# Two transfers under way: pacing GpSimd's row transfers in the first MoE layer

## The reference

```python
def reference(x, h, moe_*, moe2_*):             # cut
    # 1: causal convolution of x (4, 5696, 128) with h (5696, 128) along the sequence, by FFT
    x = irfft(rfft(x, n=2*S) * rfft(h, n=2*S)[None], n=2*S)[:, :S].reshape(22784, 128)
    # 2: MoE layer 1, 8 experts, capacity 22784 / 8 = 2848 tokens each
    logits = x @ w_gate
    for idx in argsort(-logits.flatten()):      # greedy: best (token, expert) pairs first
        tok, e = idx // 8, idx % 8
        if assigned[tok] < 0 and counts[e] < 2848: assigned[tok] = e; counts[e] += 1
    out[mask_e] = relu(x[mask_e] @ w1[e]) @ w2[e]           # 128 -> 1024 -> 128
    # 3: MoE layer 2: expert = argmax of a token's logits, no capacity
    out[mask_e] = gate_w[mask_e] * (relu(x[mask_e] @ w1b[e]) @ w2b[e])
    # gate_w: the softmax weight of the chosen expert
```

## Time and profile before

| What | Value |
|---|---|
| median of three runs | 2315.74 us |
| profiled execution: its own time; its span | 2332.93 us; 2331.1 us |
| mean granted TensorE clock | 0.919 |
| PE, DVE, ACT, POOL busy over the span | 84%, 55%, 41%, 31% |
| 743 to 1712 us (layer 1): PE, DVE, ACT, POOL busy | 781.0, 530.4, 328.1, 425.0 of 969 us |
| the same: granted clock; share of the DMA engines; GB/s | 0.91; 0.12; 35 |
| 1712 to 2331 us (layer 2): PE busy | 606.0 of 619.1 us |
| GpSimd's fetches (line 1650), 192 | median 997 ns, 941 to 2405 |
| GpSimd's sends (line 1659), 192 | median 987 ns, 968 to 1417 |
| PE idle ahead of line 828, for the fetched rows | 20.1 us in 13 places |

### The profile page before, as it was taken

One profiled execution on the slowest core, in us unless ns is written; L12 is line 12 of the kernel. 1 busy time (PEld: TensorE's weight loads), 2 busy tenths in 40 slices (PEclk: granted clock), 3 DMA queues, 4 the chain that ended last, 5 costly groups with the idle time before them and its releaser, 6 DMA issues.

```text
span 2331.1 us, 36413 instructions
## 1 busy us (share of the span) xinstructions
PE 1953.3 (84%) x10729; PEld 1517.2 (65%) x10729; DVE 1288.8 (55%) x4137; ACT 950.9 (41%) x2046; POOL 722.1 (31%) x618
## 2 busy tenths in 40 slices
PE   7886898699723988787878787987959999999998
PEld 3343444355422766565666665765759999999998
DVE  2224777422388675656666665511246666666665
ACT  2334777422111333333333232433435555555554
POOL 0001000000054344443534454345424343444434
PEclk9898999899955999998989898988979999999999
DMA  6876999787784010101110101111168888888885
GB/s 187 263 238 217 308 308 308 205 210 205 198 304 149 17 41 27 41 24 40 28 40 27 45 26 45 39 32 31 32 226 281 283 276 287 275 283 280 280 283 175
DMA packets 161018, 382.35 MB, mean 164 GB/s; under 512 B 29813, under 2 KB 88876, under 8 KB 135581
## 3 DMA queue, kind: packets, MB, share of 16 engines
q1 hardware_dynamic: 120749, 287.59, 39.1%
q10 hardware_dynamic: 11696, 57.94, 7.2%
q0 software_dynamic: 28480, 35.66, 5.4%
HBM read 273.07 MB, written 109.13 MB: 164 GB/s over the span
## 4 chain that ended last, share of the span: by engine, by line
PE 54%; issue 16%; POOL 9%; DMA 9%; DVE 7%; SPq 2%; another core or an unknown queue 1%; ACT 1%; ACTq 0%; DVEq 0%; POOLq 0%
PE bank L951 8%; PE bank L952 8%; PE bank L953 8%; POOL sorted L1659 5%; PE bank L864 5%; DMA arena<-in_dft_mid_dram 4%; POOL xr L1650 4%; PE bank L767 3%; PE bank L768 2%; DMA arena<-in_h_dram 2%; PE bank L788 2%; PE bank L688 2%; PE bank L689 2%; PE bank L750 2%; PE bank L885 2%
## 5 line engine op out<-in xcount | busy, mean ns | idle before, releaser
L1154 ACT ACTIVATE arena<-bank 128x356 f32<-128x356 f32 x512 | 239.3, 469 | 564.9 <-PE bank L887 385.3
L864 PE MATMUL bank<-arena 128*128 128x356 f32 x1024 | 407.4, 481 | 0.0
L1553 DVE SCALAR_TENSOR_TENSOR hlo<-bank,hhi 128x374 fp32r<-128x374 f32 x544 | 297.7, 548 | 192.3 <-ACT hhi L1187 132.8
L1187 ACT ACTIVATE hhi<-bank 128x374 fp32r<-128x374 f32 x544 | 263.2, 484 | 251.7 <-PE bank L953 209.1
L1687 POOL DMA_INDIRECT out_dram<-orow,slot x204 | 247.4, 1213 | 382.0 <-DVE slot L1592 324.7
L1650 POOL DMA_INDIRECT xr<-conv_y,idx x192 | 217.5, 1133 | 217.2 <-PE bank L828 144.2
L885 PE MATMUL bank<-xhi,wsp 128*128 128x356 f32 x512 | 261.5, 511 | 14.8 <-ACT arena L1154 6.3
L1659 POOL DMA_INDIRECT sorted<-arena,slot x192 | 193.7, 1009 | 164.9 <-DVE slot L1332 102.1
L951 PE MATMUL bank<-xhi,wsp 128*128 128x374 f32 x544 | 193.4, 356 | 3.3 <-DMA wsp<-w_split 3.3
L864 PEld LDWEIGHTS bank<-arena 128*128 128x128 f32 x1024 | 188.1, 197 | 0.7
L1631 POOL TENSOR_TENSOR wsp<-arena,wsp 128x1024 fp32r<-128x1024 f32 x16 | 40.4, 2530 | 469.1 <-ACT wsp L1104 469.1
(11 more groups left out here) (216 smaller groups left out, 3730.7 us busy)
## 6 DMA issues: line engine op xcount, KB each, us to landing
wsp<-w_split SPq DMA_DIRECT2D x136, 1024.0 KB, 5.3
arena<-spec_a SPq DMA_DIRECT2D x90, 320.0 KB, 3.5
spec_a<-arena ACTq DMA_DIRECT2D x16, 1600.0 KB
spec_b<-arena SPq DMA_DIRECT2D x90, 256.0 KB, 3.5
arena<-spec_b SPq DMA_DIRECT2D x16, 1280.0 KB
arena<-in_dft_mid_dram SPq DMA_DIRECT2D x90, 192.0 KB, 4.4
arena<-in_moe_w_dram SPq DMA_DIRECT2D x32, 512.0 KB, 6.3
w_split<-wsp ACTq DMA_DIRECT2D x16, 1024.0 KB, 6.3
```

The source lines that it names most:

```text
L864: r = mm(bank[Z1[t % 2]][:, 0:T1], w2raw[u][:, f * D:(f + 1) * D], h32[:, f, :], start=(f == 0), stop=(f == FC - 1))
L1154: nc.scalar.activation(h32[:, f, :], bank[H1[q % len(H1)]][:, 0:T1], ACT.Relu).then_inc(m_hh[0], 1)
L1187: nc.scalar.activation(hh[:, f, 0:T], bank[f % 4][:, 0:T], ACT.Relu).then_inc(m_hh[m_], 1)
L1553: v.scalar_tensor_tensor(hl[:, f, 0:T], bank[f % 4][:, 0:T], 0.0, hh.bitcast(F32)[:, f, 0:T], ALU.max, ALU.subtract).then_inc(m_hl[m_], 1)
```

## The change

Four things, all in layer 1. GpSimd keeps a list of the transfers under way, fetches and sends alike, and when there are two it waits for both to have landed before it asks for the next (`pace`). For that each of a tile's three transfers has a semaphore of its own, and TensorE's transpose and ScalarE's copy wait for three semaphores instead of one. `zrow` and `slot1` become one ring of eight places (a tile each; `PLACE_OF`), of the same size as the two buffers together. And `after(t)` is now t + 8 for all tiles before 51, so that behind each fetch stand the sends of the tile eight before, in an expert's first tiles as well; from tile 51 it stays t + 5, by which the sends of tiles 50 to 53 all come behind fetch 58.

```diff
+RING = 2 * GB
+PLACE = [0]
+for _i in range(1, NBT):
+    _n = BATCH[_i][1] - BATCH[_i][0]
+    _at = GB * (_i % 2) if _n == GB else PLACE[-1] + BATCH[_i - 1][1] - BATCH[_i - 1][0]
+    PLACE.append(_at if _at + _n <= RING else 0)
+PLACE_OF = {t: PLACE[BATCH_OF[t][0]] + BATCH_OF[t][1] for t in range(NT1)}
+SENT = {t: len([k for k in range(t) if PLACE_OF[k] == PLACE_OF[t]]) for t in range(NT1)}
...
             def x_T1(t):
                 u = t % 2
-                pe.wait_ge(row_ld[0][u], 48 * (t // 2 + 1))
+                for s in range(3):
+                    pe.wait_ge(row1_ld[u][s], 16 * (t // 2 + 1))
...
+                k = PLACE_OF[t]
                 if i >= 2:
                     act.wait_ge(m_oh, i - 1)
-                    if sent(i - 2, j):
-                        act.wait_ge(m_st1[i % 2][j], 48 * sent(i - 2, j))
+                for s in range(3 if SENT[t] else 0):
+                    act.wait_ge(m_st1[k][s], 16 * SENT[t])
...
+            under_way = []
+
+            def pace():
+                if len(under_way) == 2:
+                    for sem_, value in under_way:
+                        pool.wait_ge(sem_, value)
+                    under_way.clear()
+
             def fetch1(t):
...
                 for s, n in enumerate(SUBS1):
                     k = 3 * t + s
+                    pace()
+                    under_way.append((row1_ld[u][s], 16 * (t // 2 + 1)))
                     nc.gpsimd.indirect_dma_start(out=xr[u][0:n, s, 0:D], out_offset=None, in_=y_d[:, :],
-                                                 in_offset=place(idx[0:n, k:k + 1])).then_inc(row_ld[0][u], 16)
+                                                 in_offset=place(idx[0:n, k:k + 1])).then_inc(row1_ld[u][s], 16)
 
             def send1(t):
...
                 for s, n in enumerate(SUBS1):
-                    k = 3 * j + s
-                    nc.gpsimd.indirect_dma_start(out=ys_d[:, :], out_offset=place(slot1[i % 2][0:n, k:k + 1]),
-                                                 in_=zrow[i % 2][0:n, k, :], in_offset=None).then_inc(m_st1[i % 2][j], 16)
+                    k = 3 * PLACE_OF[t] + s
+                    pace()
+                    under_way.append((m_st1[PLACE_OF[t]][s], 16 * (SENT[t] + 1)))
+                    nc.gpsimd.indirect_dma_start(out=ys_d[:, :], out_offset=place(slot1[0:n, k:k + 1]),
+                                                 in_=zrow[0:n, k, :], in_offset=None).then_inc(m_st1[PLACE_OF[t]][s], 16)
...
-            def after(t):
-                if t >= PER_E * (E - 2) + 3:
-                    return t + 5
-                r = (t + 1) % PER_E
-                return t + 9 if r >= GB else t + 8 - r
-
+            after = lambda t: t + (8 if t < PER_E * (E - 2) + 3 else 5)
```

More of the change, by code:

```diff
@@ L286, in build @@
         wraw = carve(F)
-        zrow = [carve(3 * GB, ROW) for _ in range(2)]
+        zrow = carve(3 * RING, ROW)
         w2raw = [carve(F) for _ in range(2)]
@@ L357, in build @@
         slot2 = [sb(f"slot2_{i}", [P, 4], U32) for i in range(2)]
-        slot1 = [sb(f"slot1_{i}", [P, 3 * GB], U32) for i in range(2)]
+        slot1 = sb("slot1", [P, 3 * RING], U32)
         dlt = sb("dlt", [P, 24 * GB])
@@ L428, in build @@
         m_pr = sem("m_pr")
-        m_st1 = [[sem(f"m_st1{i}{j}") for j in range(GB)] for i in range(2)]
-        row_ld = [[sem(f"row_ld{m}{i}") for i in range(2)] for m in range(2)]
+        m_st1 = [[sem(f"m_st1{i}{s}") for s in range(3)] for i in range(RING)]
+        row1_ld = [[sem(f"row1_ld{i}{s}") for s in range(3)] for i in range(2)]
+        row_ld = [sem(f"row_ld{i}") for i in range(2)]
         w_ld = [[sem(f"w_ld{i}{j}") for j in range(2)] for i in range(2)]
@@ L494, in pending @@
             return found[0] if found else None
-        def sent(i, j):
-            return len([k for k in range(i % 2, i + 1, 2) if j < BATCH[k][1] - BATCH[k][0]])
         block = ctx.enter_context(nc.Block())
@@ L636, in _ @@
             sp.wait_ge(s_tab, 1)
-            for i in (NBT - 2, NBT - 1):
-                for j in range(GB):
-                    sp.wait_ge(m_st1[i % 2][j], 48 * sent(i, j))
+            for k in range(RING):
+                for s in range(3):
+                    sp.wait_ge(m_st1[k][s], 16 * len([t for t in range(NT1) if PLACE_OF[t] == k]))
             sp.wait_ge(m_pad, 16 * (E + 1))
@@ L660, in rows2 @@
                     sp.wait_ge(m_xc[1], before)
-                sp.dma_start(xr[u][:, :, :], ys_d[bass.ds(r, T3), :].rearrange("(s p) w -> p s w", p=P)).then_inc(row_ld[1][u], 16)
+                sp.dma_start(xr[u][:, :, :], ys_d[bass.ds(r, T3), :].rearrange("(s p) w -> p s w", p=P)).then_inc(row_ld[u], 16)
             rows2(sp.value_load(trow[0:1, 0:1], min_val=0, max_val=E * REGION), 0, 0)
@@ L938, in x_T @@
                 def x_T(pair, t, u):
-                    pe.wait_ge(row_ld[m_][u], 16 * (pair + 1))
+                    pe.wait_ge(row_ld[u], 16 * (pair + 1))
                     if upto(t, 1):
@@ L1134, in rows_out1 @@
                 act.wait_ge(m_zr[0], t + 1)
+                k = PLACE_OF[t]
                 if i >= 2:
                     act.wait_ge(m_oh, i - 1)
-                    if sent(i - 2, j):
-                        act.wait_ge(m_st1[i % 2][j], 48 * sent(i - 2, j))
+                for s in range(3 if SENT[t] else 0):
+                    act.wait_ge(m_st1[k][s], 16 * SENT[t])
                 copy(lgt[i % 2][:, 3 * j:3 * j + 3, :], both[:, :, D:D + E]).then_inc(m_lg, 1)
-                copy(zrow[i % 2][:, 3 * j:3 * j + 3, 0:D], both[:, :, 0:D]).then_inc(m_zrc, 1)
+                copy(zrow[:, 3 * k:3 * k + 3, 0:D], both[:, :, 0:D]).then_inc(m_zrc, 1)
             def exps1(i):
@@ L1308, in gate_onehot @@
                                 ALU.is_equal).then_inc(m_oh, 1)
-                a = 3 * BATCH[i][0]
-                own.did(v.tensor_copy(zrow[i % 2][:, 0:n, TOKCOL:TOKCOL + 1], idxf[:, a:a + n].unsqueeze(2)))
+                a, k = 3 * BATCH[i][0], 3 * PLACE[i]
+                own.did(v.tensor_copy(zrow[:, k:k + n, TOKCOL:TOKCOL + 1], idxf[:, a:a + n].unsqueeze(2)))
                 if n < 3 * GB:
@@ L1314, in gate_place @@
             def gate_place(i):
-                n = sizes[i]
+                n, k = sizes[i], 3 * PLACE[i]
                 dve.wait_ge(m_ex, i + 1)
@@ L1322, in gate_place @@
                                              added.rearrange("p e k -> p (e k)"), 0.0, ALU.mult, ALU.add))
-                own.did(v.reciprocal(zrow[i % 2][:, 0:n, GATECOL], gsum[:, 0:n]))
+                own.did(v.reciprocal(zrow[:, k:k + n, GATECOL], gsum[:, 0:n]))
                 own.wait()
@@ L1331, in gate_place @@
                 own.then(v.tensor_reduce(grank[:, 0:n], per_k(rank, n), AX, ALU.add))
-                v.tensor_copy(slot1[i % 2][:, 0:n], grank[:, 0:n]).then_inc(m_rdy[0], 1)
+                v.tensor_copy(slot1[:, k:k + n], grank[:, 0:n]).then_inc(m_rdy[0], 1)
             done = [0]
@@ L1513, in _ @@
                         own.did(v.memset(zT[u][:, T1:T3], 0.0))
-                        own.did(v.memset(zrow[u][:, :, GATECOL + 1:ROW], 0.0))
+                    own.did(v.memset(zrow[:, :, GATECOL + 1:ROW], 0.0))
                     own.did(v.memset(added[:, :, :], 0.0))
```

## The result

The changed kernel takes 2384.37 us (median of 4 runs, 2377.05 to 2386.24), the kernel before 2316.89 (4 runs) beside it: a ratio of 1.0266, interval 1.0238 to 1.0294. I had forecast 2304 us, with a range of 2268 to 2362: the sign is wrong and the time lies outside. The medians are 67.5 us apart. The profiled execution took 2383.61 us, its span is 2381.8, the mean granted clock 0.916 (before 0.919); the profiled execution of the kernel before was 16 us above that kernel's median, so the two spans are only 50.7 us apart. From the first row transpose (tile 0) to the last (tile 63) it is 968.2 us, before 919.5: 48.7 of the 50.7 us lie in this stretch.

A forecast was written before the change was run, and what follows sets the result against it. The prediction took a closed loop of TensorE, VectorE and ScalarE, clocked by the fetched rows' transposes, to bound layer 1. Its terms, 1.3 + 54 + 19.6 - 87 = -12 us, gave 2304 us as a median, range 2268 to 2362.

The forecast's parts named there:

- A pair then takes 1.3 + 2.7 = 4.0 us: GpSimd's paced requests in layer 1: two transfers, including the wait for landing, take 4.0 us, against 2.6 unpaced.
- Switch: First tiles after each expert switch: sends behind each fetch make the loop 10.8 us late, five times, plus 54 us.
- Last tiles: From tile 48 on, GpSimd at 12.0 us a tile is the bound, not TensorE at 9.7: plus 19.6 us.
- Late completions: Unnamed ScalarE and VectorE waits in long runs of GpSimd's transfers, 97 us; nine tenths go: minus 87 us.
- First tiles: At the start of layer 1, tile 0's third request waits for the first two: plus 1.3 us.
- Ring and split semaphores: Shared row places and three semaphores at TensorE's transposes and ScalarE's copies: between 0 and 3 us, taken as 0.
- A: Rival: layer 1's late completions follow the sends, not the runs; four tenths go: +36, 2352 us; chance 0.30.
- B: Rival: GpSimd sees landings sooner, a pair takes 3.6 us; all late completions gone: -58, 2258 us; chance 0.13.
- C: Rival: GpSimd's runs don't cause the late waits, so only the price is left: +75, 2391 us; chance 0.12.
- The rule of the Trainium skill: Each DMA engine goes round robin between queues, a packet at a time, so runs are no cause; pacing gives nothing back.

The follow-up runs named there:

- the window: Changed kernel with the old send order, GpSimd waiting only for the older of two transfers under way: 2191.58 us, 1.0013; again 2195.43, 1.0054.
- the early fetch: Kernel before, but GpSimd fetches a new expert's first two tiles ahead of its weight split, first expert excepted: 2170.1 us, ratio 0.9914.

## Why the prediction was wrong

**"A pair then takes 1.3 + 2.7 = 4.0 us": the step that failed.** The 2.7 was the time from a fetch's request to TensorE's use of it. GpSimd's own wake-up is later: it starts again 2.1 to 2.5 us after the *end* of the second request, 3.3 us after its start (861.78 + 0.96 + 2.35 = 865.09), for sends and fetches alike. So a pair takes 4.6 to 4.65 (median 4.66). It looks like a small error, but I had named the limit it passes: "a send that lands so late that a tile takes over 13.8 us of GpSimd and it binds everywhere". Three pairs are 14.0 us. The limit itself was too high as well: the tile distance of 13.84 came from a trace with late completions, undisturbed it is 12.9.

**Switch: I took 54 us.** The mechanism held; put 4.65 into its own working and tile 9 lands at 4 x 4.65 + 2.7 = 21.3 us behind the first request, tile 10 at 7 x 4.65 + 2.7 = 35.3. Measured: 21.4 (867.98 - 846.54) and 35.8. But I let the loss end at tile 11, as later tiles had room; with 14.0 us a tile there is none. GpSimd's list fills a whole period. From its first request at 846.54 to 958.86 it works off 23 pairs, 112.3 us (4.88 each); the last pair's two requests take 2.3, the wait for the weight split's input 8.2, the split and its gap 2.1: 124.9. Tiles 8 to 48 cost 104.7 us more than undisturbed (629.0 less 524.3), 28 of it by the order alone.

**Last tiles: plus 19.6.** They cost 51.8 over the kernel before on the same chip (233.0 less 181.2). With 4.65 the prediction's own sum gives 1475.37 + 105.0 + 13.1 + 69.1 + 55.8 = 1718.4, which is +50.8. The transpose of tile 59 waits 22.7 us, where I said some 10.

**Late completions: minus 87.** Right in kind. That they belong to long runs of GpSimd's transfers is what the runs show: they go with at most two under way, by either kind of wait (by the window, tried there only with the early fetch, all but some 10 us), and stay with the ring alone and with spread sends. The size was short. Tiles 0 to 48 lost 108.6 us to them, where I had found 97 and taken 87; the last tiles another 29.9, which I counted nowhere.

**First tiles: plus 1.3.** Tile 0's transpose now starts 7.6 us after its first request, before 5.4: 2.3 more, by the same longer pair; a small term. **Ring and split semaphores: 0** (ratios of 1.0013, 1.0022 and 0.9975) holds. Layer 2 takes as long as before.

In stretches: I expected about -3, -29 and +20 us; it was -5.9, +2.8 and +51.8, together 48.7.

**The rivals.** A, late completions follow the sends, falls: the sends are all there and the waits are gone. B, a cheaper pair, falls the other way. C gave 2391 us, 7 off, for the wrong reason: it kept every late completion, and none was kept; two errors of size met. On chips without them C's premise holds and the price alone is left: +9.0%, 200 us, not its 75. The rule of the Trainium skill that stood beside it (DMA: Bandwidth & Descriptors, Queues, rings and completion order) would make pacing give nothing back; by that rule what is late can't be waiting for a whole run in another queue, and the trace doesn't agree with the consequence, as 138 us came back. Whether what is late waits in a queue at all, no run here shows.

**Open:** what holds TensorE's results or their signals back, and why in some sets only. One rival was not tested and is not small: the recording itself. In the sets with late completions the traces lack part of the semaphores' updates, 21,286 recorded for the kernel before where another set has 27,900, and 24,261 against 27,922 for the changed kernel; they are complete in the convolution and thin wherever GpSimd sends its transfers, in layer 2 as well. Each execution on record has a span and a granted clock beside its time, so none shows the kernel without a recording: the lateness may be the recording's own, or both may have one cause. The window of two was tried on such a chip only together with the early fetch. That the early fetch alone would remove the late completions was not tried there; it leaves the long runs as they are.

## What to carry to other kernels

When a queue must be kept short, let the issuer wait for the oldest transfer of a window, not for all: here two under way cost 5 to 12 us in 2190 by the one way and 155 by the other. Price a wait by the waiting engine's own resumption in a trace, not by when another engine could use the data, and where a sum ends within a few per cent of a limit, work out the case beyond it. Put what the next tiles need ahead of a wait in the issuer's list (-0.9% here), and time a change that cures a stall on more than one chip and more than once, since the stall may not be there every time.

## What the runs showed of the hardware

- The same kernel takes 2184 to 2187 us in some sets of runs, 2317 and 2339 in others. Nearly all of it lies in layer 1 (tiles 0 to 63: 781.0 and 919.5 us), in waits of up to 9.5 us during runs of six and more of GpSimd's indirect transfers. The changed kernel takes the same in both kinds (2384 and 2385 us).
- In such a wait TensorE's matmul is recorded as ended at 893.01 and its semaphore's update at 899.02; in sets without the waits no relu starts over 0.5 us after its matmul's end. The traces of sets with the waits hold 21,000 to 24,300 updates of semaphores, the others 27,900.
- GpSimd's indirect requests take 1.0 us each, some up to 2.2, with 0.3 between them; GpSimd sees the last one's landing 3.3 us after its start, while TensorE had used rows 2.75 us after it. Emptied after each pair the queue takes a request every 2.3 us, after each three one every 2.0; a window of two lets one through every 1.6.
